# Top-k attention with a Mish MLP behind it: a block's MLP placed in four slots instead of ten, and the softmax divisor worked out later in its slot

## The chip, the cores and the metric

The kernel runs on one core of a Trainium2 chip. The metric is device time of one execution, in microseconds (us); lower is better.

## What is computed

```python
# attention: q, k, v are (4, 8, 576, 64) float32
scores = 0.125 * q @ k.T
kth    = 32nd largest of each row of scores
scores = where(scores >= kth, scores, -1e9)
attn   = exp(scores - rowmax)
attn   = attn / (sum(attn) + 1e-9)
x      = (attn @ v) as (2304, 512)
# MLP: w_in (512, 2048), w_out (2048, 512)
h = x @ w_in
g = h * tanh(softplus(h))        # Mish
y = g @ w_out
```

## The kernel before

The 2304 tokens are 18 blocks of 128 rows. The 8 heads of a block are worked on two at a time, a *duo*, so that there are 72 duos, four for each block. Two blocks, the 5th and the 14th, are mixed: they gather the last 64 rows of two batches each, and their matmuls have other shapes.

Each engine has its program written out by hand as a loop over slots, and semaphores tie the engines together. An engine takes its instructions strictly in the order of its own program. In slot s the parts of several duos are worked on at once:

- TensorE (PE): the transposes of duo s-3 (`transposes`, L332), in every even slot the two `values` products (probabilities by v, L357) of duos s-4 and s-3, the `scores` of duo s+2 (L314).
- VectorE (DVE): `topk(s)`, 8 searches for the eight largest (L558, L573) and 6 replacements (L565) on 128x576 tiles. In its midst stands `inverse(s-2)` (L548), the reciprocal of the softmax sums of duo s-2.
- ScalarE (ACT): `copy_pT` (L473), `penalties` of duo s-1 (L456), `split_q`, `copy_x` of duo s+2 from PSUM (L445), `exps` of duo s-1 with the row sums (L464).
- GpSimd (POOL): `negate` of duo s-1 (limit and maximum, once `topk(s-1)` has ended), `normalise` of duo s-2 (probabilities times reciprocal, L635), `exponents` of duo s-1 (L624), `split_q`, and `guard` of duo s-1 (adds eps to the sums, L628).

The transposes and the scores share one PSUM tile, `ps_s`. So the scores of slot s wait for ACT's copy of the transposes, and the transposes of a slot wait for the copy of the scores of the slot ahead. The transposes also wait for `normalise` of their duo, which POOL runs one slot earlier.

The MLP of a block is four up groups (16 matmuls each into `ps_u`, L373), a copy of each to `g_raw` (`copy_up`, L491), Mish in place in two halves (L498), a split of each half into a high and a low part by POOL (`split_g`, L608 and L610) and four down groups of 12 matmuls into `ps_y` (L386). Before the change each slot has one up group, from slot 6 on, and one down group, from slot 12 on. Both halves of Mish run at the end of one slot, and POOL's two `split_g` in the two slots after it. Block m thus has its up groups in slots 6+4m to 9+4m and its down groups in slots 12+4m to 15+4m. What is left after slot 74 is written behind the loop.

Of the kernel before, what the change touches and what calls it, by code (L numbers as in the profile page):

```python
# [21 lines left out]
GROUPS = 4  # L22
# [19 lines left out]
UP_SLOT, MISH_SLOT, DOWN_SLOT = 6, 10, 12  # L42
# [61 lines left out]
STAGED = PPB  # L104

# [9 lines left out]
def program(nc, k_in, q_in, v, w_in, w_out, y_out):  # L115
    with ExitStack() as ctx:
# [78 lines left out]
        glo_ready = sem("glo_ready")  # L195
        down_ready = sem("down_ready")
# [24 lines left out]
        def _(sp):  # L221
# [53 lines left out]
            for s in range(DUOS + DOWN_SLOT):  # L275
# [12 lines left out]
                m, j = divmod(s - DOWN_SLOT, GROUPS)  # L288
                if j == GROUPS - 1 and 0 <= m < BLOCKS:
                    store(m)  # L290
# [3 lines left out]
        def _(pe):  # L294
# [82 lines left out]
            def down(m, j):  # L377
# [4 lines left out]
                if j % 2 == 0:  # L382
                    pe.wait_ge(glo_ready, 2 * m + j // 2 + 1)
# [8 lines left out]
            for s in range(-2, DUOS + LAG_PT):  # L392
                if s >= LAG_PT:
                    transposes(s - LAG_PT)
                m, j = divmod(s - DOWN_SLOT, GROUPS)
                if m >= 0:
                    down(m, j)
                for d in (s - LAG_PT - 1, s - LAG_PT):
                    if d >= 0 and values_slot(d) == s:
                        values(d)  # L400
                if s + 2 < DUOS:
                    scores(s + 2)
                m, j = divmod(s - UP_SLOT, GROUPS)
                if m >= 0:
                    up(m, j)
            down(BLOCKS - 3, 3)
            for j in range(1, GROUPS):
                up(BLOCKS - 1, j)
            for j in range(GROUPS):
                down(BLOCKS - 2, j)  # L410
            for j in range(GROUPS):
                down(BLOCKS - 1, j)

        @block.scalar
        def _(act):
# [67 lines left out]
            def copy_up(m, j):  # L483
                n = GROUPS * m + j
                act.wait_ge(up_ready, n + 1)
                if n == 0:
                    act.wait_ge(wlo_ready, WCHUNKS)
# [6 lines left out]
            def mish(m):  # L494
                for h in range(2):
                    act.wait_ge(up_copied, GROUPS * m + 2 * h + 2)
                    g = g_raw[:, FT // 2 * h:FT // 2 * h + FT // 2, :]
                    act.activation(g, g, ACT.Mish).then_inc(mish_ready, 1)  # L498
# [10 lines left out]
            for s in range(-2, DUOS + LAG_PT):  # L509
                if s >= LAG_PT:  # L510
                    copy_pT(s - LAG_PT)
# [4 lines left out]
                m, j = divmod(s - UP_SLOT - 1, GROUPS)  # L516
                if m >= 0:
                    copy_up(m, j)
                if s >= LAG_PT and (s - LAG_PT) % PPB == PPB - 1:
                    copy_xT((s - LAG_PT) // PPB)  # L520
# [184 lines left out]
```

## Time and profile before

| | us |
|---|---|
| median of three runs | 783.37 (782.77 to 784.12) |
| the profiled execution's own time | 782.78 |
| its span in the trace | 781.0 |
| PE busy | 717.6 |
| DVE busy | 700.3 |
| ACT busy | 546.1 |
| POOL busy | 546.3 |

The span is what the trace shows from the first to the last instruction; the time of that execution is 1.8 us above it. Busy times are sums over the span and say nothing on who waits for whom.

### The profile page before, as it was taken

How to read it: one execution, taken by the hardware profiler on the slowest of the kernel's cores; microseconds unless marked ns; L12 is line 12 of the kernel's file. 1: busy time of each engine (PE TensorE's matmuls, PEld its weight loads, DVE VectorE, ACT ScalarE, POOL GpSimd, SP SyncE). 2: the span in 40 equal slices, each digit the busy share in tenths (PEclk: the TensorE clock that was granted, in tenths of full speed). 3: DMA queues.
4: the chain of work that ended last, by engine and by line, in shares of the span. 5: the costliest groups of instructions: out<-in, count | busy, mean ns of one | idle time of the engine just before them, and what ended most of it. 6: DMA issues, size and time to landing. Idle time of an engine off the chain costs nothing.

```text
span 781.0 us, 16741 instructions
## 1 busy us (share of the span) xinstructions
PE 717.6 (92%) x6280; PEld 641.7 (82%) x6280; DVE 700.3 (90%) x1513; ACT 546.1 (70%) x994; POOL 546.3 (70%) x677
## 2 busy tenths in 40 slices
PE   2257759999999999999999999999999999999998
PEld 2246758988888888888888888988888888889896
DVE  6999999998999999999999999998999999996000
ACT  4677666776868687878686878686868686867420
POOL 3977568697767676887676768687767776767333
PEclk9987999999999999999999999999999999999999
DMA  9521000031121000211100000020122000000000
GB/s 346 185 62 34 8 8 12 15 115 40 59 85 45 8 22 10 52 38 54 42 23 8 23 8 21 16 77 23 56 75 90 8 22 8 21 2 14 2 14 28
DMA packets 22689, 34.64 MB, mean 44 GB/s; under 512 B 2384, under 2 KB 11600, under 8 KB 22096
## 3 DMA queue, kind: packets, MB, share of 16 engines
q1 hardware_dynamic: 22608, 33.56, 13.4%
q8 instruction: 50, 0.82, 0.4%
q14 instruction: 31, 0.25, 0.1%
HBM read 28.84 MB, written 4.72 MB: 43 GB/s over the span
## 4 chain that ended last, share of the span: by engine, by line
PE 55%; DVE 32%; POOL 4%; ACT 4%; issue 4%; DMA 1%; SPq 0%; ACTq 0%; POOLq 0%
PE ps_u L373 22%; PE ps_y L386 16%; DVE left L565 15%; DVE top L573 12%; PE ps_s L314 5%; PE ps_s L332 5%; PE ps_o L357 5%; DVE top L558 5%; POOL p_sb L624 1%; PE ps_o L350 1%; ACT p_sb L464 1%; POOL g_lo L610 1%; ACT pT L473 1%; POOL p_sb L635 1%; POOL k_lo L588 1%
## 5 line engine op out<-in xcount | busy, mean ns | idle before, releaser
L573 DVE MAX8 top<-left 128x8 f32<-128x576 f32 x432 | 305.2, 751 | 0.0
L373 PE MATMUL ps_u<-xT,win 128*128 128x128 f32 x2304 | 275.6, 278 | 2.6 <-ACT xT L481 2.6
L373 PEld LDWEIGHTS ps_u<-xT,win 128*128 128x128 f32 x2304 | 263.9, 192 | 13.0 <-issue 9.2
L565 DVE MATCH_REPLACE8 left<-top,left 128x576 f32<-128x576 f32 x288 | 212.5, 748 | 0.0
L624 POOL TENSOR_TENSOR p_sb<-x_sb,p_sb 128x576 f32<-128x576 f32 x144 | 200.8, 1416 | 0.0
L464 ACT ACTIVATE p_sb<-p_sb,neg_max 128x576 f32<-128x576 f32 x144 | 111.3, 775 | 62.0 <-POOL p_sb L624 61.5
L635 POOL TENSOR_SCALAR p_sb<-p_sb,recip 128x576 f32<-128x576 f32 x144 | 106.2, 748 | 51.0 <-DVE recip L548 51.0
L386 PE MATMUL ps_y<-w_hi,g_hi 128*128 128x512 f32 x288 | 119.0, 413 | 0.7 <-ACT y_sb L504 0.7
L445 ACT ACTIVATE x_sb<-ps_s 128x576 f32<-128x576 f32 x144 | 85.6, 648 | 48.0 <-PE ps_s L314 47.8
L386 PE MATMUL ps_y<-w_hi,g_lo 128*128 128x512 f32 x288 | 113.0, 392 | 0.0
L386 PE MATMUL ps_y<-w_lo,g_hi 128*128 128x512 f32 x288 | 112.3, 390 | 0.0
L456 ACT ACTIVATE p_sb<-x_sb,limit 128x576 f32<-128x576 f32 x144 | 103.5, 770 | 8.2 <-POOL limit L615 8.2
L565 DVE MATCH_REPLACE8 left<-top,x_sb 128x576 f32<-128x576 f32 x144 | 106.3, 749 | 0.0
L558 DVE MAX8 top<-x_sb 128x8 f32<-128x576 f32 x144 | 101.4, 748 | 3.0 <-ACT x_sb L445 3.0
L473 ACT ACTIVATE pT<-ps_s 128x512 f32<-128x512 f32 (+1 forms) x144 | 84.6, 638 | 23.3 <-PE ps_s L332 23.3
L332 PE MATMUL ps_s<-ident,p_sb 128*128 128x128 f32 x648 | 85.7, 279 | 8.8 <-POOL p_sb L635 7.6
L610 POOL TENSOR_TENSOR g_lo<-g_raw,g_hi 128x1024 fp32r<-128x1024 f32 x36 | 86.0, 2389 | 3.1
L357 PEld LDWEIGHTS ps_o<-pT,v_sb 128*64 128x64 f32 x1280 | 72.0, 141 | 18.1 <-issue 13.7
L357 PE MATMUL ps_o<-pT,v_sb 128*64 128x128 f32 x1280 | 80.9, 282 | 6.1 <-ACT pT L473 6.1
L332 PEld LDWEIGHTS ps_s<-ident,p_sb 128*128 128x128 f32 x648 | 75.2, 144 | 10.4 <-ACT x_sb L445 5.9
L314 PE MATMUL ps_s<-k_hi,q_hi 64*128 64x288 f32 (+1 forms) x288 | 43.1, 362 | 42.1 <-ACT pT L473 21.4
L314 PEld LDWEIGHTS ps_s<-k_hi,q_hi 64*128 64x128 f32 (+1 forms) x288 | 25.5, 199 | 60.4 <-issue 43.6
(41 smaller groups left out, 730.1 us busy)
## 6 DMA issues: line engine op xcount, KB each, us to landing
v_sb<-v_in SPq DMA_DIRECT2D x32, 320.0 KB, 3.6
g_raw<-w_out SPq DMA_DIRECT2D x8, 512.0 KB, 3.8
win<-w_in SPq DMA_DIRECT2D x4, 1024.0 KB, 11.8
y_out<-y_sb SPq DMA_DIRECT2D x16, 256.0 KB, 2.0
k_raw<-k_in SPq DMA_DIRECT2D x14, 288.0 KB, 2.9
q_raw<-q_in SPq DMA_DIRECT2D x60, 64.0 KB, 1.8
q_raw<-q_in SPq DMA_DIRECT2D x8, 128.0 KB, 2.1
p_sb<-k_in SPq DMA_DIRECT2D x2, 288.0 KB, 5.2
```

Source lines behind the costliest of these rows:

```text
L314: mm = pe.matmul(ps_s[:, t, h, 0:HALF], q[r, s % QS, c:c + P], k[r, g % PPB, HALF * h:HALF * h + HALF], start=first, stop=final, skip_grou ...
L332: mm = pe.transpose(flat[:, P * k:P * k + P], p[:, P * k:P * k + P], ident[:, :])
L357: mm = pe.matmul(ps_o[D * h:D * h + D, j, :], v_sb[:, j, k, D * h:D * h + D], pT[:, s % 2, SPLIT_AT * h + k, :], start=(k == 0), stop=(k = ...
L373: mm = pe.matmul(ps_u[:, n % 2, i, :], win[:, k, P * f:P * f + P], xT[:, k, :], start=(k == 0), stop=(k == KC - 1), skip_group_check=True)
L386: mm = pe.matmul(ps_y[:, :], g[:, f, :], w[:, f, :], start=(f == 0 and g is g_hi and w is w_hi), stop=(f == FT - 1 and g is g_lo), skip_gr ...
L456: act.activation(p_sb[:, s % PS_, t, :], x_sb[:, s % XS, t, :], ACT.Relu, bias=limit[:, s % TS, t:t + 1], scale=-BLOW_UP).then_inc(penalty ...
L464: act.activation(p, p, ACT.Exp, bias=neg_max[:, s % TS, t:t + 1], scale=SCALE, accum_out=denom[:, s % TS, t:t + 1]).then_inc(exp_ready, 1)
L558: dve.max(best[:, t, 0:EIGHT], x[t]).then_inc(top8_ready, 1)
L565: dve.match_replace(out=left[:, t, :], in_to_replace=best[:, t, EIGHT * r:EIGHT * r + EIGHT], in_values=x[t] if r == 0 else left[:, t, :], ...
L573: dve.max(best[:, t, EIGHT * r + EIGHT:EIGHT * r + 2 * EIGHT], left[:, t, :]).then_inc(found, 1)
L624: pool.tensor_tensor(p, x_sb[:, s % XS, t, :], p, ALU.subtract).then_inc(arg_ready, 1)
L635: pool.tensor_scalar(p, p, recip[:, s % TS, t:t + 1], 1.0, ALU.mult, ALU.mult).then_inc(p_ready, 1)
```

## The change

A block's MLP now lies in four slots, here called its first to fourth slot, 6+4m to 9+4m. PE has the up groups 0 and 1 at the end of the first; up group 2 (ahead of the scores) and 3 (behind them) in the second; down group 0 at the end of the third; down group 1 ahead of the scores, 2 and 3 behind them in the fourth. ACT runs Mish on half 0 at the end of the second slot, on half 1 in the third, ahead of `copy_x`. POOL's `split_g` of half 0 is in the third slot, that of half 1 in the fourth; for the last block DVE does the second. `copy_xT` and `copy_y` move within the slot. Apart from the MLP, `guard` goes from the end of POOL's slot to the next slot, behind `negate` and `split_g`; `normalise` goes behind `exponents`; DVE's reciprocal goes from behind its first pair of replacements to behind its second.

```diff
--- before.py
+++ after.py
@@ -39,7 +39,9 @@
 BLOW_UP = 2.0 ** 90
 NEG = -3.0e38
 
-UP_SLOT, MISH_SLOT, DOWN_SLOT = 6, 10, 12
+
+
+MLP_SLOT, MLP_SLOTS = 6, 4
 WCHUNKS = 8
 FPW = FT // WCHUNKS
 
@@ -102,6 +104,15 @@
 
 
 STAGED = PPB
+
+
+def mlp_at(s):
+
+    m, r = divmod(s - MLP_SLOT, MLP_SLOTS)
+    return (m if 0 <= m < BLOCKS else None), r
+
+
+SLOTS = MLP_SLOT + MLP_SLOTS * BLOCKS
 
 
 def w_chunks_at(s):
@@ -285,8 +298,8 @@
                     for i in range(1, len(V_USES[pr])):
                         if values_slot(V_USES[pr][i - 1][3]) == s:
                             load_v(pr, i)
-                m, j = divmod(s - DOWN_SLOT, GROUPS)
-                if j == GROUPS - 1 and 0 <= m < BLOCKS:
+                m, r = mlp_at(s - 1)
+                if m is not None and r == 3:
                     store(m)
             sp.wait_ge(y_stored, 16 * stores(BLOCKS - 1))
 
...
@@ -379,7 +392,9 @@
                     pe.wait_ge(wlo_ready, WCHUNKS)
                 if j == 0 and m >= 1:
                     pe.wait_ge(y_copied, m)
-                if j % 2 == 0:
+                if j == 2 and m == BLOCKS - 1:
+                    pe.wait_ge(glo_last, 1)
+                elif j % 2 == 0:
                     pe.wait_ge(glo_ready, 2 * m + j // 2 + 1)
                 for f in range(FPG * j, FPG * j + FPG):
                     for g, w in ((g_hi, w_hi), (g_hi, w_lo), (g_lo, w_hi)):
@@ -389,27 +404,31 @@
                 mm.then_inc(down_ready, 1)
 
             pe.wait_ge(ident_ready, 1)
-            for s in range(-2, DUOS + LAG_PT):
-                if s >= LAG_PT:
+            for s in range(-2, SLOTS):
+                m, r = mlp_at(s)
+                if LAG_PT <= s < DUOS + LAG_PT:
                     transposes(s - LAG_PT)
-                m, j = divmod(s - DOWN_SLOT, GROUPS)
-                if m >= 0:
-                    down(m, j)
+
+
+                if m is not None and r == 1:
+                    up(m, 2)
+                if m is not None and r == 3:
+                    down(m, 1)
                 for d in (s - LAG_PT - 1, s - LAG_PT):
-                    if d >= 0 and values_slot(d) == s:
+                    if 0 <= d < DUOS and values_slot(d) == s:
                         values(d)
                 if s + 2 < DUOS:
                     scores(s + 2)
-                m, j = divmod(s - UP_SLOT, GROUPS)
-                if m >= 0:
-                    up(m, j)
-            down(BLOCKS - 3, 3)
-            for j in range(1, GROUPS):
-                up(BLOCKS - 1, j)
-            for j in range(GROUPS):
-                down(BLOCKS - 2, j)
-            for j in range(GROUPS):
-                down(BLOCKS - 1, j)
+                if m is not None and r == 0:
+                    up(m, 0)
+                    up(m, 1)
+                if m is not None and r == 1:
+                    up(m, 3)
+                if m is not None and r == 2:
+                    down(m, 0)
+                if m is not None and r == 3:
+                    down(m, 2)
+                    down(m, 3)
 
         @block.scalar
         def _(act):
@@ -483,19 +502,19 @@
             def copy_up(m, j):
                 n = GROUPS * m + j
                 act.wait_ge(up_ready, n + 1)
-                if n == 0:
-                    act.wait_ge(wlo_ready, WCHUNKS)
+                if m == 0 and j % 2 == 0:
+
+                    act.wait_ge(wlo_ready, WCHUNKS - 1 + j // 2)
                 if j % 2 == 0 and m >= 1:
 
                     act.wait_ge(glo_ready, 2 * (m - 1) + j // 2 + 1)
                 act.activation(g_raw[:, FPG * j:FPG * j + FPG, :], ps_u[:, n % 2, :, :],
                                ACT.Copy).then_inc(up_copied, 1)
 
-            def mish(m):
-                for h in range(2):
-                    act.wait_ge(up_copied, GROUPS * m + 2 * h + 2)
-                    g = g_raw[:, FT // 2 * h:FT // 2 * h + FT // 2, :]
-                    act.activation(g, g, ACT.Mish).then_inc(mish_ready, 1)
+            def mish(m, h):
+                act.wait_ge(up_copied, GROUPS * m + 2 * h + 2)
+                g = g_raw[:, FT // 2 * h:FT // 2 * h + FT // 2, :]
+                act.activation(g, g, ACT.Mish).then_inc(mish_ready, 1)
 
             def copy_y(m):
                 act.wait_ge(down_ready, GROUPS * m + GROUPS)
@@ -506,23 +525,29 @@
             split_k(0)
             split_q(0)
             split_k(1)
-            for s in range(-2, DUOS + LAG_PT):
-                if s >= LAG_PT:
+            for s in range(-2, SLOTS + 1):
+                m, r = mlp_at(s)
+                if LAG_PT <= s < DUOS + LAG_PT:
                     copy_pT(s - LAG_PT)
                 if 0 <= s - LAG_EXP < DUOS:
                     penalties(s - LAG_EXP)
                 if s + 3 < DUOS:
                     split_q(s + 3)
-                m, j = divmod(s - UP_SLOT - 1, GROUPS)
-                if m >= 0:
-                    copy_up(m, j)
-                if s >= LAG_PT and (s - LAG_PT) % PPB == PPB - 1:
-                    copy_xT((s - LAG_PT) // PPB)
+                if m is not None and r == 0:
+                    copy_xT(m)
+                if m is not None and r == 1:
+                    copy_up(m, 1)
+                    if s >= DUOS + LAG_PT:
+                        mish(m, 0)
+                    copy_up(m, 2)
+                if m is not None and r == 2:
+                    copy_up(m, 3)
+                    mish(m, 1)
                 if 0 <= s + 2 < DUOS:
                     copy_x(s + 2)
-                m, j = divmod(s - DOWN_SLOT, GROUPS)
-                if m >= 0 and j == GROUPS - 1:
-                    copy_y(m)
+                before, last = mlp_at(s - 1)
+                if before is not None and last == 3:
+                    copy_y(before)
                 if 0 <= s - LAG_EXP < DUOS:
                     exps(s - LAG_EXP)
                 if s > -2:
@@ -530,16 +555,10 @@
                         split_k(g)
                 for c in w_chunks_at(s):
                     split_w(c)
-                m, j = divmod(s - MISH_SLOT, GROUPS)
-                if m >= 0 and j == 0:
-                    mish(m)
-            copy_up(BLOCKS - 1, 0)
-            copy_y(BLOCKS - 3)
-            for j in range(1, GROUPS):
-                copy_up(BLOCKS - 1, j)
-            mish(BLOCKS - 1)
-            copy_y(BLOCKS - 2)
-            copy_y(BLOCKS - 1)
+                if m is not None and r == 0:
+                    copy_up(m, 0)
+                if m is not None and r == 1 and s < DUOS + LAG_PT:
+                    mish(m, 0)
 
         @block.vector
         def _(dve):
@@ -566,7 +585,7 @@
                                           in_to_replace=best[:, t, EIGHT * r:EIGHT * r + EIGHT],
                                           in_values=x[t] if r == 0 else left[:, t, :],
                                           imm_value=NEG).then_inc(found, 1)
-                    if r == 0 and s >= LAG_NORM:
+                    if r == 1 and s >= LAG_NORM:
                         inverse(s - LAG_NORM)
                     for t in range(2):
                         dve.wait_ge(found, 12 * s + 4 * r + 1 + t)
@@ -581,6 +600,14 @@
             for s in range(DUOS - LAG_NORM, DUOS):
                 inverse(s)
 
+            g, f = BLOCKS - 1, slice(FT // 2, FT)
+            dve.wait_ge(mish_ready, 2 * g + 2)
+            dve.wait_ge(down_ready, GROUPS * g)
+            dve.tensor_copy(g_hi[:, f, :], g_raw[:, f, :]).then_inc(ghi_last, 1)
+            dve.wait_ge(ghi_last, 1)
+            dve.tensor_tensor(g_lo[:, f, :], g_raw[:, f, :], g_hi[:, f, :].bitcast(F32),
+                              ALU.subtract).then_inc(glo_last, 1)
+
         @block.gpsimd
         def _(pool):
             def split_k(g):
@@ -641,28 +668,27 @@
                                pattern=[[-1, P]], channel_multiplier=1).then_inc(ident_ready, 1)
             split_q(0)
             split_k(1)
-            for s in range(-2, DUOS + LAG_NORM):
+            for s in range(-2, SLOTS):
+                m, r = mlp_at(s)
                 if 0 <= s - LAG_EXP < DUOS:
                     negate(s - LAG_EXP)
-                m, j = divmod(s - MISH_SLOT - 1, GROUPS)
-                if m >= 0 and j < 2:
-                    split_g(m, j)
+                if m is not None and r == 2:
+                    split_g(m, 0)
+                if m is not None and r == 3 and m < BLOCKS - 1:
+                    split_g(m, 1)
                 for c in w_chunks_at(s - 1):
                     split_w(c)
-                if 0 <= s - LAG_NORM:
-                    normalise(s - LAG_NORM)
+                if 0 <= s - LAG_NORM < DUOS:
+                    guard(s - LAG_NORM)
                 if 0 <= s - LAG_EXP < DUOS:
                     exponents(s - LAG_EXP)
+                if 0 <= s - LAG_NORM < DUOS:
+                    normalise(s - LAG_NORM)
                 if s + 3 < DUOS:
                     split_q(s + 3)
-                if 0 <= s - LAG_EXP < DUOS:
-                    guard(s - LAG_EXP)
                 if s > -2:
                     for g in splits_at(s):
                         split_k(g)
-            for m in range(BLOCKS - 2, BLOCKS):
-                for h in range(2):
-                    split_g(m, h)
 
 
 def kernel(q, k, v, moe_w_in, moe_w_out):
```

POOL's program in a slot in which it splits a half of g, before the change (in order of issue; L615 and L617 are `negate`, L608 and L610 `split_g`, L635 `normalise`, L624 `exponents`, L628 `guard`):

```order
L615 TENSOR_SCALAR limit<-top 128x2
L617 TENSOR_SCALAR neg_max<-top 128x2
L608 CAST g_hi<-g_raw 128x1024
L610 TENSOR_TENSOR g_lo<-g_raw,g_hi 128x1024
L635 TENSOR_SCALAR p_sb<-p_sb,recip 128x576 x2
L624 TENSOR_TENSOR p_sb<-x_sb,p_sb 128x576 x2
L594 TENSOR_TENSOR q_lo<-q_raw,q_hi 128x128
L628 TENSOR_SCALAR denom<-denom 128x2
```

And POOL's program in the third slot of a block after it (L642 and L644 are `negate`, L635 and L637 `split_g`, L655 `guard`, L651 `exponents`, L662 `normalise`):

```order
L642 TENSOR_SCALAR limit<-top 128x2
L644 TENSOR_SCALAR neg_max<-top 128x2
L635 CAST g_hi<-g_raw 128x1024
L637 TENSOR_TENSOR g_lo<-g_raw,g_hi 128x1024
L655 TENSOR_SCALAR denom<-denom 128x2
L651 TENSOR_TENSOR p_sb<-x_sb,p_sb 128x576 x2
L662 TENSOR_SCALAR p_sb<-p_sb,recip 128x576 x2
L621 TENSOR_TENSOR q_lo<-q_raw,q_hi 128x128
```

`normalise` stood directly behind `split_g` and now stands behind `guard` and `exponents` too.

ACT's program around Mish before the change, from the copy of the scores in one slot to the exponentials of the next (L445 `copy_x`, L464 `exps`, L498 Mish, L473 `copy_pT`, L456 `penalties`, L491 `copy_up`):

```order
L445 ACTIVATE x_sb<-ps_s 128x576 x2
L464 ACTIVATE p_sb,denom<-p_sb,neg_max 128x576 x2
L498 ACT_TABLE_LOAD
L498 ACTIVATE g_raw<-g_raw 128x1024 x2
L473 ACTIVATE pT<-ps_s 128x512
L473 ACTIVATE pT<-ps_s 128x640
L456 ACTIVATE p_sb<-x_sb,limit 128x576 x2
L434 ACTIVATE q_hi<-q_raw 128x128
L491 ACTIVATE g_raw<-ps_u 128x512
L445 ACTIVATE x_sb<-ps_s 128x576 x2
L504 ACTIVATE y_sb<-ps_y 128x512
L464 ACT_TABLE_LOAD
```

After it, from the up copies of a block's second slot to the exponentials of its third (L511 `copy_up`, L464 `copy_x`, L483 `exps`, L517 Mish, L492 `copy_pT`, L475 `penalties`):

```order
L464 ACTIVATE x_sb<-ps_s 128x576 x2
L483 ACTIVATE p_sb,denom<-p_sb,neg_max 128x576 x2
L517 ACT_TABLE_LOAD
L517 ACTIVATE g_raw<-g_raw 128x1024
L492 ACTIVATE pT<-ps_s 128x512
L492 ACTIVATE pT<-ps_s 128x640
L475 ACTIVATE p_sb<-x_sb,limit 128x576 x2
L453 ACTIVATE q_hi<-q_raw 128x128
L511 ACTIVATE g_raw<-ps_u 128x512
L517 ACTIVATE g_raw<-g_raw 128x1024
L464 ACTIVATE x_sb<-ps_s 128x576 x2
L483 ACT_TABLE_LOAD
```

The second half of Mish has moved behind the transposes' copies, the penalties and the last up copy; the number of table loads is as before, two in a block.

## Rows read from the trace of the kernel before

**Rows 1.** The page: span, and busy time of each engine (share of the span).

```profile
span 781.0 us, 16741 instructions
PE 717.6 (92%) x6280; PEld 641.7 (82%) x6280; DVE 700.3 (90%) x1513; ACT 546.1 (70%) x994; POOL 546.3 (70%) x677
```

**Rows 2.** The chain that ended last: start us, us, what.

```profile
159.50 1.83 PE ps_s L314 x12
...
611.05 2.77 PE ps_y L386 x12
...
744.46 10.72 PE ps_u L373 x96
...
766.75 11.19 PE ps_y L386 x48
```

**Rows 3.** Timeline of PE, slot 62: start us, us, line, instruction, [idle before].

```profile
618.42 1.15 PE L332 MATMUL ps_s<-ident,p_sb 128*128 128x128 f32 x9
...
622.26 2.40 PE L357 MATMUL ps_o<-pT,v_sb 128*64 128x128 f32 x40
624.60 0.53 PE L314 MATMUL ps_s<-k_hi,q_hi 64*128 64x288 f32 x4
...
625.59 3.84 PE L373 MATMUL ps_u<-xT,win 128*128 128x128 f32 x32
629.26 1.15 PE L332 MATMUL ps_s<-ident,p_sb 128*128 128x128 f32 x9
```

**Rows 4.** Timeline of DVE: the starts of two duos' searches.

```profile
66.14 1.40 DVE L558 MAX8 top<-x_sb 128x8 f32<-128x576 f32 x2
...
75.84 1.40 DVE L558 MAX8 top<-x_sb 128x8 f32<-128x576 f32 x2
```

**Rows 5.** The waits of the span: us in total, times, longest us.

```profile
DVE recip L548 <- POOL denom L628: 19.2, 7, 9.3
```

**Rows 6.** Timeline of ACT, slots 62 and 63.

```profile
625.69 1.19 ACT L445 ACTIVATE x_sb<-ps_s 128x576 f32<-128x576 f32 x2 [0.38 <-PE ps_s L314]
626.77 0.78 ACT L464 ACTIVATE p_sb<-p_sb,neg_max 128x576 f32<-128x576 f32 x1
...
628.19 0.20 ACT L464 ACTIVATION_READ_ACCUMULATOR p_sb<-p_sb,neg_max 128x1 f32 x1
628.41 1.28 ACT L498 ACT_TABLE_LOAD   x1
629.70 2.02 ACT L498 ACTIVATE g_raw<-g_raw 128x1024 f32<-128x1024 f32 x2
```

**Rows 7.** Timeline of POOL, slot 63.

```profile
630.83 1.04 POOL L608 CAST g_hi<-g_raw 128x1024 fp32r<-128x1024 f32 x1 [1.24 <-ACT g_raw L498]
...
634.34 1.48 POOL L635 TENSOR_SCALAR p_sb<-p_sb,recip 128x576 f32<-128x576 f32 x2
635.78 2.79 POOL L624 TENSOR_TENSOR p_sb<-x_sb,p_sb 128x576 f32<-128x576 f32 x2
638.52 0.46 POOL L594 TENSOR_TENSOR q_lo<-q_raw,q_hi 128x128 fp32r<-128x128 f32 x1
640.29 0.22 POOL L628 TENSOR_SCALAR denom<-denom 128x2 f32<-128x2 f32 x1 [1.31 <-ACT p_sb L464]
```

**Rows 8.** Timelines of POOL (slot 5) and PE (slot 6), near the start.

```profile
59.46 1.47 POOL L635 TENSOR_SCALAR p_sb<-p_sb,recip 128x576 f32<-128x576 f32 x2
...
61.08 2.15 PE L332 MATMUL ps_s<-ident,p_sb 128*128 128x128 f32 x9 [2.23 <-POOL p_sb L635]
...
66.75 2.40 PE L357 MATMUL ps_o<-pT,v_sb 128*64 128x128 f32 x20 [1.18 <-ACT pT L473]
...
70.48 3.84 PE L373 MATMUL ps_u<-xT,win 128*128 128x128 f32 x32
```

**Rows 9.** Timeline of POOL: the two splits of k in one slot.

```profile
167.84 2.81 POOL L588 TENSOR_TENSOR k_lo<-k_raw,k_hi 128x576 fp32r<-128x576 f32 x2 [0.34 <-ACT k_hi L424]
```

**Rows 10.** Timeline of PE: scores and up group behind a long wait.

```profile
117.62 0.70 PE L314 MATMUL ps_s<-k_hi,q_hi 64*128 64x288 f32 x4 [4.76 <-ACT pT L473]
...
119.22 4.78 PE L373 MATMUL ps_u<-xT,win 128*128 128x128 f32 x32
```

More of the change, by code:

```diff
@@ L195, in program @@
         glo_ready = sem("glo_ready")
+        ghi_last = sem("ghi_last")
+        glo_last = sem("glo_last")
         down_ready = sem("down_ready")
@@ L274, in _ @@
                 sp.dma_start(win[:, k, :], w_in[P * k:P * k + P, :]).then_inc(win_loaded, 16)
-            for s in range(DUOS + DOWN_SLOT):
+            for s in range(SLOTS + 1):
                 if STAGED < s + 3 < DUOS:
```

## The prediction

> **What bounds the kernel now.** I read the page first: PE is busy 92% of the span and DVE 90%, ACT and POOL 70% [rows 1]. Two engines that full can't both have much to give. The chain of waits says which counts where: it lies on DVE at first and then mostly on PE, to the end, with transposes, down, values, scores and up groups back to back; its last pieces are up and down groups alone [rows 2]. The starts of the searches are 9.70 us apart [rows 4], so 38.8 us for a block's four slots. For PE I take each piece from start to start: a down group 2.77 us [rows 2]; transposes and a down group together 618.42 to 622.26 = 3.84, so the transposes 1.07; two values products 2.34; scores 0.99; an up group 3.67 [rows 3]. An up group that follows another is 10.72/3 = 3.57 [rows 2]. Four slots are 4 x (1.07 + 2.77 + 0.99 + 3.67) + 2 x 2.34 = 38.7 us. PE and DVE are level to 0.1 us in a block; PE has no room for a wait.
>
> DVE waits for its reciprocal 19.2 us in all, 9.3 of them once, behind its last search [rows 5]. The 9.9 us ahead of it fall where POOL splits g and k in one slot. Behind the last search PE still has up and down groups of three blocks; its last down groups end at 766.75 + 11.19 = 777.94 [rows 2], 3.06 us before the end of the span, for the copy of y and its store.
>
> **What the change gives.** The instructions are nearly the same; their places are new. The work of block 16 and a group of each kind leave the tail, since down groups start in slot 8 and not in slot 12. Priced alone: PE would be short of work for four slots fewer of down groups and lose less at the end. Also no g split falls into the slots with two k splits (14, 15, 50, 51), so DVE's waits there should go. The cover for all this is PE's own time, so I follow PE through a block and look for new waits.
>
> **The second and third slot, step by step.** Time 0 is PE's transposes in the block's second slot.
> - PE: transposes to 1.07, up group 2 to 4.74, scores to 5.73, up group 3 to 9.40. There the third slot begins.
> - ACT copies the scores 625.69 - 624.60 = 1.09 after they start [rows 3, 6], at 5.83. The exponentials follow 1.08 later, at 6.91 (their arguments are ready before, since POOL has no g split in this slot). From their start to the table load it is 1.64, from there to Mish 1.29, and from Mish to POOL's cast 630.83 - 629.70 = 1.13 [rows 6, 7]. So the cast of half 0 starts at 6.91 + 1.64 + 1.29 + 1.13 = 10.97, that is 1.57 us into the third slot.
> - POOL has stood at this cast since `negate`, and behind it stand `guard`, `exponents` and `normalise`. `split_g` takes 634.34 - 630.83 = 3.51, to 14.48; `guard` 0.22; `exponents` 638.52 - 635.78 = 2.74; `normalise` 1.48 [rows 7]: 18.92. From its end to the transposes it is 61.08 - 60.93 = 0.15 [rows 8]. The fourth slot's transposes start at 19.07.
> - PE's own work in the third slot is 1.07 + 2.34 + 0.99 + 2.77 = 7.17, to 16.57. It waits 19.07 - 16.57 = 2.50 us, in up to three pieces: ACT is in Mish when the transposes are done, so the values wait some 0.4; down group 0 starts late by 0.3, since `split_g` ends at 14.48; the rest, 1.8, ahead of the transposes.
>
> Before the change the same row of waits did no harm: `normalise` came directly behind `split_g`, 5.1 us after the transposes of the slot (629.26 to 634.34), and PE had 8.5 us of work in the slot [rows 3, 7]. Now the slot with the least work on PE, 7.2 us, has the longest row on POOL, and `exponents` stand ahead of `normalise`.
>
> The fourth slot: half 1 went through Mish in the third, so `split_g` follows POOL's q split and ends some 4.2 us in, before down group 2 wants it at 1.07 + 2.77 + 0.99 = 4.83. The slot is PE's work, 1.07 + 0.99 + 3 x 2.77 = 10.37. The first: 1.07 + 2.34 + 0.99 + 3.57 + 3.67 = 11.64; ACT and POOL are done before it ends. The block takes 19.07 + 10.37 + 11.64 = 41.1 us, 2.3 more than DVE's pace. DVE can't use its lead: its reciprocal now waits in the third slot for `guard`, which ends at 14.70, so it is held to the same 41.1.
>
> Here the Trainium skill has another price for a term ("ScalarE: Activation LUTs", What ACT_TABLE_LOAD costs): a switch of tables costs the load and a drain of about 1.38 us. The row shows the load starting at 628.41, with the accumulator read ahead of it done at 628.39, and Mish starting as the load ends [rows 6]. No drain shows; an estimate by the page would put 1.38 on the row of waits in each block, 23 us over 17 of them. By the row it is nothing, and I go by the row.
>
> **The sum.** POOL's `normalise` in slot 5 starts at 59.46 [rows 8]; with `guard` and `exponents` ahead of it the transposes of slot 6 start at 59.46 + 0.22 + 2.74 + 1.48 + 0.15 = 64.05. The way to the first up group took 70.48 - 61.08 - 1.18 = 8.2 us at the low clock [rows 8], and two up groups 7.24: the first block's second slot starts at 79.5. Sixteen blocks of 41.1 bring 657.6: 737.1.
>
> Extras: in the mixed blocks scores take 1.83 instead of 0.99 [rows 2, 3]; it counts in three of four slots, 2.5 a block, 5.0 for both. In slots 15 and 51, second slots, two k splits (2.81 us [rows 9]) stand on POOL ahead of the g split, and their ACT copies ahead of Mish: I take 1.6 each, and 0.7 each for slots 31 and 32, 4.6 in all. These are my reckoning; zero and 10 are their bounds. Less 1.0 for the scores that slot 70 has no more. The second slot of block 16 starts at 745.7.
>
> Without scores the row of waits there is 1.5 shorter, 17.6; the fourth slot 9.4: 772.7. Block 17: transposes and values 3.4, the copy of xT 0.7, four up groups 14.5, four down groups 11.1, Mish and splits hidden behind up 2, 3 and down 0, 1: 802.4. With 3.06 for y the span is 805.5, the execution's own time 1.8 more, 807.3. The median of before is 0.6 above its profiled execution; I predict **807** against 783.4, 3% slower. It is a balance of two terms: waits of 16 x 2.5 in the third slots, 3.0 in that of block 16 and 4.6 behind k splits, less 1.7 for mixed scores that then would count, in all 45.9; and what the layout gives without them, 781.0 - (805.5 - 45.9) = 21.4.
>
> **Rivals.**
> - *PE sets the pace and the change does what its layout suggests (faster, 0.11).* For it: all work fits, 38.7 a block, and the order lets PE run ahead in other slots. It needs the wait of 2.50 gone: 805.5 - 45.9 = 759.6, as a median 762. It decides where the wait is 1.1: (807 - 783.4)/17 = 1.4 less than mine. Against it: the row of waits is all durations, and no link has slack, as POOL is idle ahead of the cast and ACT is not.
> - *Half the wait is found (about equal, 0.03).* If ACT and POOL overlap better by 1.4 us than I add up: 783.
> - *The clock falls (0.03).* Behind a wait of 4.76 us scores took 119.22 - 117.62 = 1.60 instead of 0.99, and an up group 4.78 instead of 3.84 [rows 10]. Such a loss of 1.5 in each of 17 blocks gives 832. My longest wait is 1.8.
> - *A table switch costs more than its row (0.02).* If Mish started 1.38 later behind the load, the row of waits is that much longer: 807 + 17 x 1.38 = 830. It is the case of the page named above; the row speaks against it.
>
> **The numbers.** The forecast has 0.81, with 790 to 824: a wait 0.7 shorter or longer in 17 blocks is 12 us, and the extras' bounds and the clock at the start lie inside. The clock in slot 6 could rise sooner (3 us less) or two up groups run slowly (4 each more). The range is the same, and leaves out all four rivals, 0.19; to take in the half wait would widen it by 7 us for 0.03. Differences under 0.2% can't be told from none. Slower: 0.81 + 0.05 for the two dear rivals = 0.86; the half wait goes to same, 0.02, and slower, 0.01: 0.87; faster 0.11.
>
> **What the profile after would show.** Right: the waits name PE's transposes on POOL's `normalise`, about 1.8 us in each block, and POOL's cast on ACT's Mish; DVE's reciprocal waits for `guard`, some 2.3 us a block, 35 to 40 in all; the up groups of one block start 41.1 us after those of the last; PE busy falls to near 90% in the middle. Wrong: blocks 38.8 apart, with POOL's cast never waiting; and if the blocks are 41 apart but PE waits elsewhere, the row of waits is not the one I follow.

## The result

The changed kernel takes 807.62 us (median, 807.37 to 808.89) against 783.62 before: a ratio of 1.0311, 95% interval 1.0293 to 1.0329. It is 3.1% slower. The profiled execution's span is 805.4 us, 24.4 above that of before.

The page of the changed kernel, against [rows 1]:

```profile
span 805.4 us, 16744 instructions
PE 719.0 (89%) x6280; PEld 642.6 (80%) x6280; DVE 703.2 (87%) x1515; ACT 554.4 (69%) x996; POOL 547.5 (68%) x675
```

Busy times have hardly moved. What is new is idle time, and the waits of the changed kernel say where (us in total, times, longest):

```profile
POOL p_sb L651 <- ACT p_sb L475: 109.9, 33, 5.0
DVE recip L567 <- POOL denom L655: 58.7, 19, 8.0
POOL g_hi L635 <- ACT g_raw L517: 57.9, 16, 18.5
...
PE ps_s L345 <- POOL p_sb L662: 46.9, 21, 6.8
...
PE ps_o L370 <- ACT pT L492: 6.6, 14, 1.4
PE ps_y L401 <- POOL g_lo L637: 5.7, 14, 1.3
```

PE now waits for `normalise` (L662) ahead of its transposes (L345) 46.9 us, against 7.6 before. That row of the page of before:

```profile
L332 PE MATMUL ps_s<-ident,p_sb 128*128 128x128 f32 x648 | 85.7, 279 | 8.8 <-POOL p_sb L635 7.6
```

In the timeline, 28.7 of the 46.9 us lie ahead of the 17 fourth slots, 1.7 each; the other 18.2 lie ahead of slots 3 to 6, before the MLP begins. So the 46.9 is not the prediction's sum of waits, 45.9, which it happens to be near. DVE's wait for `guard`, 19.2 before [rows 5], is 58.7. The chain that ended last in the changed kernel, in the block of slots 58 to 61 (start us, us, what), from the scores of its second slot to the transposes of its fourth; pieces of 0.07 us and less are left out:

```profile
627.02 1.04 PE ps_s L327 x12
...
628.16 0.44 issue
628.60 0.64 ACT x_sb L464
629.24 1.51 ACT p_sb L483 x4
...
630.76 1.28 ACT L517
...
632.06 1.07 ACT g_raw L517
...
633.18 1.05 POOL g_hi L635
634.31 2.38 POOL g_lo L637
636.69 0.08 issue
636.77 0.22 POOL denom L655
636.99 0.08 issue
637.07 2.83 POOL p_sb L651 x2
639.90 1.47 POOL p_sb L662 x2
641.37 0.14 issue
641.51 1.17 PE ps_s L345 x9
```

It leaves PE at the scores, goes over ACT (copy, exponentials, table load, Mish) and POOL (split, eps, exponents, normalise) and comes back 14.5 us later. PE in the meantime, in the timeline of the same stretch:

```profile
631.62 1.15 PE L345 MATMUL ps_s<-ident,p_sb 128*128 128x128 f32 x9
632.70 1.31 PE L370 MATMUL ps_o<-pT,v_sb 128*64 128x128 f32 x20
634.34 1.31 PE L370 MATMUL ps_o<-pT,v_sb 128*64 128x128 f32 x20 [0.33 <-ACT pT L492]
...
641.51 1.17 PE L345 MATMUL ps_s<-ident,p_sb 128*128 128x128 f32 x9 [1.71 <-POOL p_sb L662]
```

The third slot, 631.62 to 641.51, is 9.89 us long for 7.17 us of work by the prediction's count. From the starts of the transposes of every slot one gets the lengths of slots and blocks. In a block that is regular throughout, slots 42 to 45, and the start of the next:

```profile
442.35 1.14 PE L345 MATMUL ps_s<-ident,p_sb 128*128 128x128 f32 x9
...
454.00 1.15 PE L345 MATMUL ps_s<-ident,p_sb 128*128 128x128 f32 x9
...
463.31 1.15 PE L345 MATMUL ps_s<-ident,p_sb 128*128 128x128 f32 x9
...
473.21 1.17 PE L345 MATMUL ps_s<-ident,p_sb 128*128 128x128 f32 x9 [1.67 <-POOL p_sb L662]
...
483.61 1.14 PE L345 MATMUL ps_s<-ident,p_sb 128*128 128x128 f32 x9
```

The tables here and below hold such lengths. A *regular* block has no mixed tiles, on its own or its neighbours' account, and no k splits (the splits of a new batch's k into a high and a low part); there are ten, and the block of slot 6, where the clock has just risen, is not one of them.

| us | first | second | third | fourth | regular block | blocks with slots 15, 31, 51 |
|---|---|---|---|---|---|---|
| changed kernel | 11.65 | 9.31 | 9.90 | 10.40 | 41.26 | 44.4, 43.2, 44.4 |

Before, such blocks take 38.72 us, as from 618.42 [rows 3] to the transposes four slots on; slots start at other places of the MLP there:

```profile
657.14 1.15 PE L332 MATMUL ps_s<-ident,p_sb 128*128 128x128 f32 x9
```

### The profile page after: what moved, and what is told of

Its sections match the earlier page's. It is cut to its first block, busy times and chain, and to the rows that moved or that the text cites. A ratio compares the mean times of both kernels' runs of the same rounds, so it can differ in the third digit from the quotient of the medians.

```text
span 805.4 us, 16744 instructions
## 1 busy us (share of the span) xinstructions
PE 719.0 (89%) x6280; PEld 642.6 (80%) x6280; DVE 703.2 (87%) x1515; ACT 554.4 (69%) x996; POOL 547.5 (68%) x675
## 3 DMA queue, kind: packets, MB, share of 16 engines
q1 hardware_dynamic: 22608, 33.56, 12.9%
## 4 chain that ended last, share of the span: by engine, by line
PE 62%; POOL 19%; ACT 9%; DVE 6%; issue 3%; DMA 0%; SPq 0%; ACTq 0%; POOLq 0%
PE ps_u L386 25%; PE ps_y L401 19%; PE ps_s L345 7%; PE ps_s L327 7%; POOL p_sb L651 6%; POOL g_lo L637 5%; PE ps_o L370 5%; POOL p_sb L662 3%; ACT p_sb L483 3%; DVE left L584 3%; ACT L517 2%; POOL g_hi L635 2%; DVE top L592 2%; ACT g_raw L517 2%; ACT x_sb L464 1%
## 5 line engine op out<-in xcount | busy, mean ns | idle before, releaser
L651 POOL TENSOR_TENSOR p_sb<-x_sb,p_sb 128x576 f32<-128x576 f32 x144 | 202.5, 1428 | 112.9 <-ACT p_sb L475 109.9
L386 PE MATMUL ps_u<-xT,win 128*128 128x128 f32 x2304 | 268.6, 276 | 1.4 <-ACT xT L500 1.4
L492 ACT ACTIVATE pT<-ps_s 128x512 f32<-128x512 f32 (+1 forms) x144 | 86.0, 647 | 123.5 <-PE ps_s L345 123.2
L345 PE MATMUL ps_s<-ident,p_sb 128*128 128x128 f32 x648 | 87.0, 282 | 46.9 <-POOL p_sb L662 46.9
L483 ACT ACTIVATE p_sb<-p_sb,neg_max 128x576 f32<-128x576 f32 x144 | 110.9, 775 | 19.6 <-POOL p_sb L651 18.0
L401 PE MATMUL ps_y<-w_hi,g_hi 128*128 128x512 f32 x288 | 116.9, 406 | 6.0 <-POOL g_lo L637 5.7
L345 PEld LDWEIGHTS ps_s<-ident,p_sb 128*128 128x128 f32 x648 | 75.8, 145 | 56.9 <-issue 54.7
L464 ACT ACTIVATE x_sb<-ps_s 128x576 f32<-128x576 f32 x144 | 85.6, 646 | 47.4 <-PE ps_s L327 47.4
L662 POOL TENSOR_SCALAR p_sb<-p_sb,recip 128x576 f32<-128x576 f32 x144 | 106.6, 752 | 0.3 <-DVE recip L567 0.3
L475 ACT ACTIVATE p_sb<-x_sb,limit 128x576 f32<-128x576 f32 x144 | 103.2, 769 | 0.5 <-POOL limit L642 0.5
L637 POOL TENSOR_TENSOR g_lo<-g_raw,g_hi 128x1024 fp32r<-128x1024 f32 x35 | 83.8, 2394 | 3.0
L635 POOL CAST g_hi<-g_raw 128x1024 fp32r<-128x1024 f32 x35 | 36.4, 1040 | 57.9 <-ACT g_raw L517 57.9
L401 PEld LDWEIGHTS ps_y<-w_hi,g_hi 128*128 128x128 f32 x288 | 54.0, 188 | 21.3 <-issue 9.9
```

The lines of the kernel that those rows point to most:

```text
L345: mm = pe.transpose(flat[:, P * k:P * k + P], p[:, P * k:P * k + P], ident[:, :])
L386: mm = pe.matmul(ps_u[:, n % 2, i, :], win[:, k, P * f:P * f + P], xT[:, k, :], start=(k == 0), stop=(k == KC - 1), skip_group_check=True)
L401: mm = pe.matmul(ps_y[:, :], g[:, f, :], w[:, f, :], start=(f == 0 and g is g_hi and w is w_hi), stop=(f == FT - 1 and g is g_lo), skip_gr ...
L475: act.activation(p_sb[:, s % PS_, t, :], x_sb[:, s % XS, t, :], ACT.Relu, bias=limit[:, s % TS, t:t + 1], scale=-BLOW_UP).then_inc(penalty ...
L483: act.activation(p, p, ACT.Exp, bias=neg_max[:, s % TS, t:t + 1], scale=SCALE, accum_out=denom[:, s % TS, t:t + 1]).then_inc(exp_ready, 1)
L637: pool.tensor_tensor(g_lo[:, f, :], g_raw[:, f, :], g_hi[:, f, :].bitcast(F32), ALU.subtract).then_inc(glo_ready, 1)
```

## The experiments

All kernels were timed against the kernel before on the same chip. Times are medians; the interval is that of the ratio to the kernel before (783.0 to 783.9 in these comparisons).

**The layout alone** (`e1_layout`): the four slots, with `guard`, `normalise` and the reciprocal as before.

```diff
-                    if r == 1 and s >= LAG_NORM:
+                    if r == 0 and s >= LAG_NORM:
                         inverse(s - LAG_NORM)
...
                 if 0 <= s - LAG_NORM < DUOS:
-                    guard(s - LAG_NORM)
+                    normalise(s - LAG_NORM)
                 if 0 <= s - LAG_EXP < DUOS:
                     exponents(s - LAG_EXP)
-                if 0 <= s - LAG_NORM < DUOS:
-                    normalise(s - LAG_NORM)
                 if s + 3 < DUOS:
                     split_q(s + 3)
+                if 0 <= s - LAG_EXP < DUOS:
+                    guard(s - LAG_EXP)
```

> The MLP in four slots, but guard, normalise and the reciprocal where they were before the change. Theory (the third slot's row of waits on ACT and POOL): normalise now comes directly behind split_g, so PE's 1.7 us ahead of the fourth slot's transposes go. But exponents come 1.4 us later, so the exponentials, the next transposes' copy and with it the fourth slot's scores come later, and guard at the end of POOL's slot holds the second split_g until the exponentials are done: down group 2 waits about 2 us. Block 41 to 42 us, total 805 to 820: undoing this half alone gains nothing. Rival (the later guard and reciprocal are what costs, the four slots are sound): PE's work sets the pace, blocks of 38.8 us, total about 762 to 770.

Measured: 832.45, ratio 1.0625 (1.0603 to 1.0647), 25 us slower than the whole change. The third slot fell to 8.05 as expected, but the fourth rose to 12.9 in some blocks and, in ten of the 17, 1.6 higher still (14.5 in a regular one). One of the longer kind, in its timeline of PE:

```profile
489.79 0.54 PE L327 MATMUL ps_s<-k_hi,q_hi 64*128 64x288 f32 x4 [0.20 <-ACT pT L492]
...
492.97 0.50 PE L401 MATMUL ps_y<-w_hi,g_hi 128*128 128x512 f32 x1 [2.12 <-POOL g_lo L637]
...
493.54 0.40 PE L401 MATMUL ps_y<-w_hi,g_lo 128*128 128x512 f32 x1
493.78 0.52 PE L401 MATMUL ps_y<-w_hi,g_hi 128*128 128x512 f32 x1
494.10 0.63 PE L401 MATMUL ps_y<-w_lo,g_hi 128*128 128x512 f32 x1
```

PE waits 2.12 us for the second `split_g`, which is the wait expected; and soon after it some down matmuls take 0.63 instead of 0.40 us. The granted clock is 0.88 over this fourth slot, and in its second half, in the windows view (stretch, length, busy time of PE, granted clock, DMA share, GB/s):

```profile
493.00:500.00 7.00, 7.00 (x24) 0.76 0.03 9
```

That second part was not foreseen; it costs 1.6 us in each block where it comes. The wait itself is that of `guard` at the end of POOL's slot: it stands 110.3 us in this kernel for the exponentials, 72 times. The direction of the theory holds; its size (805 to 820) missed the clock. The rival, 762 to 770, is out: the four slots by themselves are the slower part.

**The order alone** (`e2_order`): the kernel before, with the new order of `guard`, `exponents`, `normalise` and the later reciprocal.

```diff
-                if 0 <= s - LAG_NORM:
-                    normalise(s - LAG_NORM)
+                if 0 <= s - LAG_NORM < DUOS:
+                    guard(s - LAG_NORM)
                 if 0 <= s - LAG_EXP < DUOS:
                     exponents(s - LAG_EXP)
+                if 0 <= s - LAG_NORM < DUOS:
+                    normalise(s - LAG_NORM)
...
-                if 0 <= s - LAG_EXP < DUOS:
-                    guard(s - LAG_EXP)
```

> The kernel before, with guard, normalise and the reciprocal moved as in the change, the MLP in its ten slots. Theory: in the slot with the first split_g the row split_g, guard, exponents, normalise ends about 9.6 us after the slot's transposes, where PE has 8.5 us of work: about 1.1 us of wait in each block, 0 to 18 us in all since the DVE waits behind the k splits (9 us) shrink: 780 to 800. Rival (the reordering by itself only removes DVE's waits): 9 us less, about 775.

Measured: 802.85, ratio 1.0247 (1.0230 to 1.0264), 3 us beyond the expected range. In its timeline of PE, a slot with the first `split_g`:

```profile
439.98 1.15 PE L332 MATMUL ps_s<-ident,p_sb 128*128 128x128 f32 x9
...
449.86 1.17 PE L332 MATMUL ps_s<-ident,p_sb 128*128 128x128 f32 x9 [1.20 <-POOL p_sb L635]
```

The slot takes 9.88 us instead of 8.51, and regular blocks 40.06 instead of 38.72. The 1.3 us, where 1.1 was expected, comes in every block. DVE's wait for the reciprocal doesn't shrink either; it is 34.4 us in all, against 19.2. Each half of the change is slower by itself; together they are better than the layout alone, since the new order takes `guard`'s wait for the exponentials off the second `split_g`.

**Guard ahead of the split** (`e3_guard`).

```diff
+                if 0 <= s - LAG_NORM < DUOS:
+                    guard(s - LAG_NORM)
                 if m is not None and r == 2:
                     split_g(m, 0)
...
-                if 0 <= s - LAG_NORM < DUOS:
-                    guard(s - LAG_NORM)
```

> The changed kernel with guard ahead of split_g on POOL. Theory: DVE's wait for the reciprocal (2.5 us in the third slot of each block) goes nearly to zero and DVE runs ahead, but PE's row of waits loses only guard's own 0.3 us: 16 x 0.3, about 803. Rival (DVE's wait for the reciprocal sets the pace): 16 x 2.5 less, about 768.

Measured: 802.29, ratio 1.0237 (1.0222 to 1.0253), as the theory had it; regular blocks 40.83. DVE's wait didn't go to zero but to 48.5 us: with the hold in the third slot nearly gone (0.42 us in the block looked at) DVE runs ahead and waits in the next slot (1.43). Had DVE's wait set the pace, the total would have fallen to about 768. So DVE doesn't set the pace of these blocks.

**Mish of half 0 early** (`e4_mish0`).

```diff
                 if m is not None and r == 1:
                     copy_up(m, 1)
-                    if s >= DUOS + LAG_PT:
-                        mish(m, 0)
+                    mish(m, 0)
                     copy_up(m, 2)
...
-                if m is not None and r == 1 and s < DUOS + LAG_PT:
-                    mish(m, 0)
```

> The changed kernel with Mish of half 0 directly behind the second up copy in the second slot, as the last block has it; this costs two more table loads a block on ACT. Theory: the cast of half 0 then starts when POOL is free, about 2.5 to 3 us earlier, split_g is over before the third slot's penalties are done, and PE waits some 0.4 us in place of 2.5 in the third slot: 16 x 2.1 less, about 774, faster than the kernel before. Rival (the two more table loads, 2.6 us a block, delay ACT and by it PE as much as is gained): 800 or more.

Measured: 791.16, ratio 1.0096 (1.0081 to 1.0111): the right direction, half the size. Regular blocks are 39.68, 1.58 shorter, not 2.1 (the third slot falls by 1.85, to 8.05, and the fourth grows by 0.27), and the blocks with k splits in their second slot are longer: 46.2, 45.1 and 46.2. The timeline of POOL in the first of these:

```profile
165.81 0.73 POOL L618 TENSOR_TENSOR q_lo<-q_raw,q_hi 128x256 fp32r<-128x256 f32 x1
170.49 2.77 POOL L612 TENSOR_TENSOR k_lo<-k_raw,k_hi 128x576 fp32r<-128x576 f32 x2 [3.94 <-ACT k_hi L443]
173.34 0.22 POOL L639 TENSOR_SCALAR limit<-top 128x2 f32<-128x2 f32 x1
173.65 0.21 POOL L641 TENSOR_SCALAR neg_max<-top 128x2 f32<-128x2 f32 x1
173.81 1.04 POOL L632 CAST g_hi<-g_raw 128x1024 fp32r<-128x1024 f32 x1
```

ACT's copy of k stands behind the exponentials, which now have a table load ahead of them; POOL waits 3.94 us for it, and the g split stands behind.

**More work on POOL, in two places** (`e5_pad3`, `e6_pad1`). Four small copies that nothing reads.

```diff
+        spare = sb("spare", [P, 32])
...
+                if m == 0 and r == 0:
+                    pool.wait_ge(win_loaded, 16 * KC)
...
+                if m is not None and r == 2:       # e6_pad1: r == 0, ahead of split_g
+                    pool.wait_ge(spare_done, m)
+                    for i in range(4):
+                        cp = pool.tensor_copy(spare[:, 8 * i:8 * i + 8], win[:, 0, 8 * i:8 * i + 8])
+                    cp.then_inc(spare_done, 1)
```

> The changed kernel with four small copies (nothing reads them) on POOL behind split_g in each third slot, about 1.1 to 1.2 us in all. Theory: POOL's row ahead of the fourth slot's transposes is on the path in every block, so the total grows by the copies' whole length times 17: 19 us, about 827. Rival (POOL's queue there has slack, PE or DVE sets the pace): under 4 us more.

> The same four copies on POOL in each first slot, where POOL waits 2.6 us for the penalties. Theory: covered, within 1.5 us of 807.6. Rival (any work added to POOL costs): as much as in the third slot, about 827.

Measured: 828.74 in the third slot (ratio 1.0580, 1.0563 to 1.0598), 807.69 in the first (1.0313, 1.0298 to 1.0329). Place decides, as expected. But the 21 us in the third slot agree with the 19 expected by accident. The copies overlap and delay what follows by 0.50, not 1.15: third slots take 10.40 instead of 9.90, 8.5 us in 17 blocks. The rest comes from fourth slots that are 1.6 us longer, in 7 of the 17 blocks (12.0 instead of 10.4 in regular ones), 11.2 us in all, and from the first MLP slot, 1.4 longer at a granted clock of 0.80 instead of 0.88. One fourth slot of either kind, in the windows view of that kernel (stretch, length, busy time of PE, PEld, DVE, ACT and POOL, then the granted clock, DMA share and GB/s):

```profile
399.70:410.10 10.40, 10.37 (x57) 8.50 (x58) 10.40 (x23) 5.70 (x12) 9.72 (x14) 1.00 0.03 9
441.50:453.50 12.00, 12.00 (x58) 9.67 (x58) 12.00 (x27) 5.54 (x12) 9.68 (x14) 0.86 0.04 12
```

The same matmuls, 1.6 us longer at a granted clock of 0.86. With the wait 0.5 us longer than in the changed kernel the clock falls in these 7 blocks, and in an eighth, that of slots 30 to 33, whose fourth slot (12.0, granted clock 0.86) already took 11.8 in the changed kernel.

**Normalise ahead of exponents in third slots** (`e7_norm`).

```diff
+                if m is not None and r == 2 and 0 <= s - LAG_NORM < DUOS:
+                    normalise(s - LAG_NORM)
                 if 0 <= s - LAG_EXP < DUOS:
                     exponents(s - LAG_EXP)
-                if 0 <= s - LAG_NORM < DUOS:
+                if not (m is not None and r == 2) and 0 <= s - LAG_NORM < DUOS:
                     normalise(s - LAG_NORM)
```

> The changed kernel with normalise ahead of exponents in third slots only. Theory: the 1.7 us wait ahead of the fourth slot's transposes goes, but exponents end 1.5 us later, ACT's exponentials and the copy of the next transposes follow later, and the scores of the fourth slot wait about 1.4 us, down group 2 some 0.6 more: the wait moves, 0.3 us a block is left of the gain, 800 to 806. Rival (normalise being late is the whole cost): 16 x 1.7 less, about 780.

Measured: 808.45 (1.0318, 1.0302 to 1.0333). The third slot falls by 1.84, to 8.06, and the fourth rises by 1.6, to 12.0: the wait moves. The block of slots 30 to 33 pays more, 46.6 instead of 43.2, which takes the rest of the gain: in its fourth slot PE waits 3.29 us for the second `split_g`, and the granted clock is 0.80.

**Exponentials ahead of the copy and Mish, no more table loads** (`e8_exps`): ACT's second slot is first up copy, `exps`, `copy_x`, `mish(m, 0)`, `copy_up(m, 2)`.

> The changed kernel with ACT's second slot in the order: first up copy, exponentials, copy of the scores, Mish of half 0, second up copy; no more table loads. Theory: Mish ends about 1.2 us earlier, so does everything behind it, and the values products in the third slot no longer wait for ACT: 16 x 1.25 less, about 788. Rival (Mish's place doesn't matter, POOL's own work does): 805 or more.

Measured: 798.94 (1.0199, 1.0183 to 1.0214). Regular blocks 40.25, 1.01 shorter and not 1.25; the three with k splits are 1.3 longer each. A share of that is the clock: in their third slots PE waits 2.2 us for the first `split_g`, and the granted clock is 0.86 or 0.87, where the changed kernel has 1.00. So Mish's place is on the path, with less than I had added up.

**Towards a faster version** (`e9_k`, `e10_x`, `e11_all`, `e12_k2`), each on top of the early Mish; `e10_x` and `e11_all` also have the edit of `e9_k`.

```diff
 # e9_k, POOL: k splits of second slots at the end of the third
-                    for g in splits_at(s):
-                        split_k(g)
+                    for t in ([s - 1] if m is not None and r == 2 else []) + ([s] if r != 1 or m is None else []):
+                        for g in splits_at(t):
+                            split_k(g)
 # e10_x, ACT: copy_x(s + 2) ahead of mish(m, 1); e11_all: that and e7_norm's edit
 # e12_k2, from e9_k: those of third slots at the end of the fourth as well
+                    for t in ([s - 1] if m is not None and r >= 2 else []) + ([s] if m is None or r in (0, 3) else []):
```

> The kernel with the early Mish of half 0 (791.2), and POOL's k splits of second slots moved to the end of the next slot. Its trace shows why the early Mish gave 16 us and not 33: regular blocks fell from 41.26 to 39.68, but the three with k splits in the second slot rose from 44.4, 43.2 and 44.4 to 46.2, 45.1 and 46.2, their third slots to 13.4, 12.4 and 13.4 us. Theory: POOL stands at the k split, which waits for ACT's copy behind the exponentials, ahead of split_g; moved, the third slots fall to 8 to 10 us and the fourth rise by up to 2: 2 x 1.6 + 4 = 7 us less, about 784. Rival (ACT's k copies themselves are the delay): under 2 us less.

> The same with the copy of the scores ahead of Mish of half 1 in the third slot. Theory: with the early Mish the fourth slot's transposes wait for that copy, which stands behind a table load and Mish (the copy ends 0.1 us ahead of them); ahead of it, they wait for normalise alone, 0.35 us earlier: 16 x 0.35 less, about 779. Rival (normalise ends as late anyway): no change, 784.

> The same, and in third slots normalise ahead of exponents. Theory: the fourth slot's transposes come when PE's own work is done, third slots fall to 7.2 us, blocks to about 39.0: 4 to 6 us less, about 774. Rival (as in the run with normalise moved alone, the wait moves to the scores of the fourth slot): no change or slower, 779 to 783.

> The kernel with the early Mish of half 0 and the moved k splits (787.5), and POOL's k splits of third slots moved to the end of the fourth. In its trace one block stands out, the one of slots 30 to 33: two k splits at the end of its third slot wait for ACT's late copy, the second split_g comes late, and the fourth slot takes 17.1 us in place of 10.7. Theory: with one k split there whose copy is long done the slot falls to about 11.5: 5 to 6 us less, about 782, level with or just under the kernel before. Rival (the k split only waits elsewhere): 786 to 788.

| | median | ratio, 95% interval | regular block | third, fourth slot | blocks with slots 15, 31, 51 |
|---|---|---|---|---|---|
| e9_k | 787.49 | 1.0042 (1.0028 to 1.0056) | 39.68 | 8.06, 10.66 | 43.6, 46.7, 43.6 |
| e10_x | 794.20 | 1.0136 (1.0122 to 1.0149) | 40.18 | 7.71, 11.50 | 43.6, 47.2, 43.6 |
| e11_all | 793.51 | 1.0127 (1.0114 to 1.0141) | 40.18 | 7.68, 11.54 | 43.3, 46.9, 43.3 |
| e12_k2 | 782.19 | 0.9983 (0.9974 to 0.9992) | 39.68 | 8.04, 10.67 | 43.5, 40.8, 43.6 |

`e9_k` gained in the two blocks with mixed scores (slots 14 to 17 and 50 to 53) and lost in the third, slots 30 to 33, whose third slot now had two k splits at its end: in its fourth slot PE waits 3.29 us for the second `split_g`, and the granted clock is 0.80. In `e10_x` my theory was right on the third slot (0.35 shorter) and wrong on the block: the copy now waits 0.37 us for the scores, which Mish had filled, Mish has come behind it, and the exponentials end later. The timeline of PE shows where it is paid:

```profile
473.06 0.53 PE L327 MATMUL ps_s<-k_hi,q_hi 64*128 64x288 f32 x4 [1.00 <-ACT pT L492]
```

`e10_x`, expected at about 779, came to 794. In `e11_all`, expected at about 774, the fourth slot's scores are held the same (1.07 us), and the place of `normalise` makes next to no difference. `e12_k2` came out as expected, level with the kernel before: 0.17% less, with an interval that just excludes no change, and less than the 0.2% that the prediction calls no difference. The fourth slot of the block of slots 30 to 33 fell from 17.1 to 11.2, with the long wait and the fall of the clock both gone (1.00). No other kernel here came down to the time of before.

## Why the prediction was right

- *PE can't take a wait, 38.7 us of work in a block.* No run here beat 39.68 us for a regular block in four slots, and none showed PE busy throughout one; the first two slots, which are PE's work alone, measure 11.65 and 9.31 in every variant.
- *The row of waits from the second slot's scores to the fourth's transposes.* Shown from both sides: an earlier head (e4, e8) shortens the third slot, more work in the row (e5) lengthens it by 0.50 us, and the same work in the first slot (e6) costs nothing. It starts and ends where forecast. The cast came 1.56 us into the third slot (forecast 1.57). The slot took 9.90 and not 9.67, because POOL leaves 0.08 us around `guard`, which I had at nothing, and the two exponents take 2.8. The other slots were 11.65, 9.31 and 10.40 (11.64, 9.40, 10.37); the block 41.26 (41.1). The three pieces of PE's wait were 0.33, 0.19 and 1.71 in the block looked at (0.4, 0.3, 1.8).
- *The start.* Transposes of slot 6 at 64.28 (64.05). The second slot began at 77.41 and not 79.5: the clock rose sooner, as allowed for in the range. Its granted value over slot 6 is 0.88, against 0.66 before.
- *Extras.* The sixteen blocks up to the second slot of block 16 took 668.5 (666.2 by the prediction: regular blocks 0.16 longer each, extras and the missing scores together 8.3 instead of 8.6). It began at 745.9, forecast 745.7. That the extras come so near is partly luck: the blocks of slots 14 and 50 took 3.1 more than a regular one and not 4.1, the block of slot 30 1.9 and not 1.4, and the missing scores took only 0.2 off slot 70 and not 1.0, since PE waited 0.70 us there for the copy of xT.
- *The tail.* Last down group at its end 802.35 (forecast 802.4), span 805.4 (805.5). That total is closer than its terms: the start was 2.1 us too late and the sixteen blocks 2.3 too short. The sum ends at 807.3 for the profiled execution (807.37 measured); the 0.6 by which the median of before lies above its profiled execution is named and then not added. With it the forecast would have been 808, against a median of 807.62.
- *DVE only follows.* Shown by guard ahead of the split: DVE's waits change place, and the time falls by 5.3 us, where the row of waits lost about 0.4 in a regular block. In the block looked at its reciprocal waited 2.50 us (about 2.3 forecast).
- *Signs that came out otherwise.* DVE's wait for `guard` was forecast at 35 to 40 us in all and is 58.7: it is 5.0 in each of the two blocks with k splits and mixed scores, and 6.1 and 8.0 at the end. PE busy was to fall to near 90% in the middle; it is 39.05 of the 41.26 us in a regular block, 95%, against all of the 38.72 us before. The slot lengths, not the busy share, show the wait.
- *The drain behind a table load*, which the Trainium skill prices at about 1.38 us ("ScalarE: Activation LUTs", What ACT_TABLE_LOAD costs): the changed kernel shows none either. The load starts at 630.76, 0.01 after the exponentials, and Mish at 632.06.
- *The rivals.* PE's pace (762) didn't come about. The clock's fall had 0.03 and didn't come about in this kernel; but the run with the longer wait shows it was close: behind a wait of 1.7 it falls in none of 17 blocks, behind 2.2 in 8.
- *What the layout gives without the waits, 21.4 us.* This was only reckoned. `e12_k2` took 25 us off the changed kernel, of the 45.9 us of waits forecast; the rest wasn't reached by any kernel here, so whether the layout could give 21.4 us stays open.

## What to carry to other kernels

When two engines are both near full in a steady loop, follow one period from instruction to instruction with measured durations before anything else: here a dozen durations from the trace of before gave the new period of 41.26 us to 0.2. Packing a stage into fewer slots makes light slots and heavy ones. Here the light slot's 7.2 us of PE work gained nothing, since the row of steps on ACT and POOL beside it ended 9.9 us after its start. Undoing or moving one edit in this loop mostly moved the wait (e1, e7, e10). What helped was starting the head of the row earlier, and then looking at the few irregular periods, which held all of the last 9 us.

## What the runs showed of the hardware

TensorE's clock falls behind waits shorter than the 4.76 us of the kernel before [rows 10]. In the run with the padded third slot it falls behind a wait of about 2.2 us ahead of the transposes, in 8 of 17 blocks; the granted clock is 0.84 to 0.86 in the slot, and in seven of them 1.6 us are lost. In the layout alone it falls in ten of 17 fourth slots, behind a wait of 2.1 to 3.3 us for the second `split_g`. In the changed kernel, with waits of 1.7, it stays at 1.00 from the first block's second slot on. So 0.5 us more of waiting cost 0.5 in some blocks and 2.1 in others. Why one block and not its neighbour, no run here tells.

Four copies of 128x8 in a row on POOL take 0.56 to 0.59 us together; where the trace shows one by itself, it takes 0.19. Back to back they overlap.
